# Attention on one core: eight of the fifteen maxima ahead of the first values, and the last output turned later

## The chip, the cores and the metric

The kernel runs on one core of a Trainium2 chip. A core has five engines with instruction queues of their own: TensorE (PE, matrix products, with its weight loads shown apart as PEld), VectorE (DVE), ScalarE (ACT), GpSimd (POOL) and SyncE (SP, which issues transfers). They wait for each other through semaphores alone. The metric is the time of one execution on the device in microseconds (us).

## What is computed

The whole program is an attention, a small mixture of experts on its output, and a two-layer network. The change touches the attention alone, and in it 32 heads (4 batches of 8) that all run through the same steps:

```
batch, n_heads, seq, head_dim = (4, 8, 1152, 64)
q_pool = q.reshape(B, H, S // factor, factor, D).mean(axis=3)      # factor = 2: 576 queries
scores = scale * np.matmul(q_pool, k.transpose(0, 1, 3, 2))        # 576 x 1152
scores = scores - np.max(scores, axis=-1, keepdims=True)
attn = np.exp(scores)
attn = attn / (np.sum(attn, axis=-1, keepdims=True) + 1e-09)
return np.matmul(attn, v).astype(np.float32)
```

## The kernel before

Each head's scores are computed twice. The first time is for the row maxima: 15 pieces of 128 queries by 384 keys, each one matmul (`max_piece` on TensorE, line 382) into one of two PSUM banks and one reduction on VectorE (`max_piece`, line 647). Piece n may be written only when VectorE has reduced piece n-2, since both lie in the same bank; the semaphores `max_freed0` and `max_freed1` say so. I call the pieces maximum 0 to maximum 14. When all fifteen are reduced, one short reduction (line 661) makes the row maximum out of them; it is written into the low part of the queries, which TensorE then turns (`turn_q_lo_m`, line 328 with `q_lo_m`) so that the maximum is subtracted inside the second product.

The second time is for the attention itself, transposed: nine tiles of 128 keys by 576 queries (`score`, two matmuls of line 392 and two of line 401), each followed by an exponential on ScalarE (line 576) into `pT`. Score j needs the exponential of tile j-2, since two tiles' banks alternate. The product with the values (`values`, line 415) goes tile by tile: four tiles in the middle of an iteration, five at its end. GpSimd adds tiles 0 to 6 of the exponentials (line 270), VectorE the last two and the rest (`add_late`, lines 668 to 681), which gives each query's sum.

The loop runs heads in an overlapped way. Iteration h (0 to 30) computes scores, exponentials and values of head h and, between them, the fifteen maxima of head h+1. It also turns the queries of head h+2 (`turn_queries`, line 328 with `q_hi`, four transposes), its keys (`turn_keys`: "ka", "kb" of four transposes each, "kc" of head h+1), and, of head h-1, the finished output (`turn_out`, line 426, three transposes) and its row sums (`sum_rows`, line 431). VectorE's `normalise` (lines 688 to 708, six instructions) then divides that output. Iteration 30 has no head h+2 and leaves those transposes out. The last head, 31, has no maxima beside it; its places are filled with the first steps of the experts.

The order on each engine is written out by hand in this loop; no scheduler moves anything. Engines run their queues strictly in that order. An iteration falls into a first half, from score 0 to the first values, the four tiles of values, a second half from there to `turn_q_lo_m`, and that with the last five tiles of values.

Of the kernel before, what the change touches and what calls it, by code (L numbers as in the profile page):

```python
# [53 lines left out]
def attention(nc, q, k, v, x_all, x_ready, ident, ident_r, ready, ahead):  # L54
# [49 lines left out]
    with ctx:  # L104
# [213 lines left out]
        def _(pe):  # L318
# [12 lines left out]
            def turn_keys(h, name, tiles):  # L331
                if name == "ka":
                    pe.wait_ge(k_split, h + 1)
                claim_turn((name, h))
                sources = [k_parts[h % 2][:, j, :] for j in tiles]
                if name == "kc":
                    sources.append(q_hi2[h % 2][:, QT - 1, :])
                turn_to(turn.bitcast(F32R), sources).then_inc(turned, 1)
# [47 lines left out]
            def score(h, j):  # L386
                u, n = h % 2, h * KT + j
                if n >= 2:
                    pe.wait_ge(exp_done, n - 1)
                out = scores[n % 2]  # L390
                for half in range(2):
                    nc.tensor.matmul(out[:, half, 0:HALF], kT[u][:, j * P:(j + 1) * P],  # L392
                                     qT[h % 3][:, half * HALF:(half + 1) * HALF],
                                     start=True, stop=False)
                if j == 0:
                    pe.wait_ge(k1_copied, h + 1)
                    for use in (Q_LO, Q_LO_LAST):
                        at = max_no(h, use)
                        pe.wait_ge(max_freed[at % 2], at // 2 + 1)
                for half in range(2):  # L400
                    mm = nc.tensor.matmul(out[:, half, 0:HALF], kT1[u][:, j * P:(j + 1) * P],  # L401
                                          qTm[u][:, half * HALF:(half + 1) * HALF],
                                          start=False, stop=True)
                mm.then_inc(scores_ready, 1)

            def values(h, tiles):
                u = h % 2
                if tiles[0] == 0:
                    pe.wait_ge(v_loaded[u], 16 * (h // 2 + 1))
                    pe.wait_ge(qa_copied, min(h + 3, HEADS))  # L410
                for j in tiles:
                    pe.wait_ge(exp_done, h * KT + j + 1)
                    for half in range(2):
                        at = half * SHIFT
                        mm = nc.tensor.matmul(o_bank[half * D:(half + 1) * D, at:at + HALF],  # L415
                                              v_raw[u][:, j, :],
                                              pT[:, j, half * HALF:(half + 1) * HALF],
                                              start=(j == 0), stop=(j == KT - 1))
                    mm.then_inc(pv_done, 1)

            def turn_out(h):

                pe.wait_ge(o_copied, h + 1)
                claim_turn(("out", h))
                for t in range(3):
                    nc.tensor.transpose(turn[:, t * P:(t + 1) * P], oT[:, t * P:(t + 1) * P],
                                        ident[:, :])

            def sum_rows(h):
                pe.wait_ge(groups_summed, h + 1)  # L430
                mm = nc.tensor.matmul(turn[:, 3 * P:3 * P + QT * GROUPS], all_groups[:, :],
                                      group_sums[:, :], start=True, stop=True)
                mm.then_inc(turned, 1)
# [14 lines left out]
            for h in range(HEADS - 1):  # L448
                more2 = h + 2 < HEADS

                def maxima(a, z):
                    for at in range(a, z):
                        max_piece(h + 1, at)

                score(h, 0)
                maxima(0, 2)
                turn_keys(h + 1, "kc", [KT - 1])
                score(h, 1)
                maxima(2, 3)
                score(h, 2)  # L460
                maxima(3, 4)
                if more2:
                    turn_queries(h + 2)
                maxima(4, 5)
                score(h, 3)
                maxima(5, 6)
                if h > 0:
                    turn_out(h - 1)
                maxima(6, 7)
                if h > 0:  # L470
                    sum_rows(h - 1)
                maxima(7, 8)
                score(h, 4)
                maxima(8, 9)
                values(h, range(EARLY))
                maxima(9, 11)
                score(h, 5)
                maxima(11, 12)
                if more2:
                    turn_keys(h + 2, "ka", range(0, 4))  # L480
                maxima(12, 13)
                score(h, 6)
                maxima(13, 14)
                score(h, 7)
                maxima(14, 15)
                score(h, 8)
                if more2:
                    turn_keys(h + 2, "kb", range(4, 8))
                turn_q_lo_m(h + 1)
                values(h, range(EARLY, KT))  # L490
# [6 lines left out]
            first(0, ("x", 1))  # L497
            score(h, 3)
            first(0, ("x", 2))
            turn_out(h - 1)  # L500
            sum_rows(h - 1)
            first(0, ("x", 3))
            score(h, 4)
            first(0, ("x_last",))
            values(h, range(EARLY))
            score(h, 5)
            first(0, ("qk", 0, 0))
# [135 lines left out]
        def _(dve):  # L643
# [90 lines left out]
            maximum(0)  # L734
            for h in range(HEADS - 1):
                for at in range(len(PIECES)):
                    if at == 9 and h > 0:
                        normalise(h - 1)
                    max_piece(h + 1, at)
                maximum(h + 1)  # L740
                add_late(h)

            def add_tile(j, n):

                total, h = p_sum[:, 0:SQ], HEADS - 1
                dve.wait_ge(exp_done, h * KT + j + 1 if j < KT else HEADS * KT)
                if j == KT:
                    dve.wait_ge(part_summed, h * (len(ON_POOL) - 1) + len(LAST_ON_POOL) - 1)
                if n == 0:
                    ins = nc.vector.scalar_tensor_tensor(  # L750
                        total, pT[:, LAST_ON_POOL.stop, :], EPS / P, pT[:, j, :], ALU.add, ALU.add)
                else:
                    dve.wait_ge(p_summed, h * SUM_STEPS + n)
                    ins = nc.vector.tensor_tensor(total, total, pT[:, j, :], ALU.add)
                ins.then_inc(p_summed, 1)
# [2 lines left out]
            first(0, ("x", 0))  # L758
            first(0, ("x", 1))
            first(0, ("x", 2))  # L760
            normalise(h - 1)
            first(0, ("x", 3))
            first(0, ("x_last",))
            add_tile(5, 0)
            first(0, ("qk", 0, 0))
            add_tile(6, 1)
# [1505 lines left out]
```

## Time and profile before

| | us |
|---|---|
| median of 3 runs | 1187.63 |
| lowest, highest | 1186.3, 1188.55 |
| the profiled execution | 1186.41 |
| its span, first to last instruction | 1184.6 |
| TensorE busy | 1122.5 (95%) |
| VectorE busy | 806.1 (68%) |
| GpSimd busy | 673.6 (57%) |
| ScalarE busy | 620.6 (52%) |

The profile comes from one execution. Busy time is the union of an engine's instruction records; a matmul's record includes the pipeline's fill and drain, so that a stretch can show TensorE as fully busy while it issues late. Hence the starts of the records are what to read. The attention's loop takes the first 510 us of the span. Where iterations lie in it:

| stretch, us | iterations |
|---|---|
| 38.16 to 160.76 | 1 to 8 |
| 192.40 to 208.98 | 11 |
| 242.37 to 261.84 | 14 |
| 295.47 to 494.59 | 17 to 29 |
| 494.59 to 509.74 | 30 |

Columns of the busy table by stretch: the stretch and its length; for TensorE, its weight loads, VectorE, ScalarE and GpSimd in that order the us busy and, in brackets, the instructions; the granted TensorE clock as a share of full speed; the DMA engines' busy share; GB/s.

### The profile page before, as it was taken

What the parts mean: (1) busy time and instruction counts of PE and PEld (TensorE: products, weight loads), DVE (VectorE), ACT (ScalarE), POOL (GpSimd) and SP (SyncE); (2) the same over time, 40 slices, a digit from 0 to 9 for tenths busy, and PEclk for the clock granted to TensorE, in tenths of its full rate; (3) what the DMA queues carried; (4) which work ended last, traced back from release to release, by engine and by line L of the source; (5) the groups of instructions that cost most, each with busy time, mean ns of one, the idle gap of its engine ahead of it and who ended that gap; (6) DMA issues with size and microseconds to landing.
All of it is one profiled execution on the core that took longest, in us unless ns stands there. A gap on an engine that the chain in (4) does not pass through costs nothing. (4 is left out here: it accounts for less than half of the span.)

```text
span 1184.6 us, 19899 instructions
## 1 busy us (share of the span) xinstructions
PE 1122.5 (95%) x7088; PEld 930.8 (79%) x7088; DVE 806.1 (68%) x1574; ACT 620.6 (52%) x1228; POOL 673.6 (57%) x687
## 2 busy tenths in 40 slices
PE   6999999989999999998898989789999999999998
PEld 5877777777788777787777777568888898888987
DVE  5888877767888888866556565665448754686554
ACT  4666665566666666655565656632334333443331
POOL 5888899998888888744332335503334333633330
PEclk9999999999999999998999999999999999999999
DMA  8221111211112121001001011123221522223121
GB/s 206 61 61 57 48 53 58 60 43 50 61 61 61 60 61 41 22 1 36 2 1 41 2 38 62 54 87 95 71 72 54 169 64 71 71 64 114 54 71 54
DMA packets 76593, 71.47 MB, mean 60 GB/s; under 512 B 11856, under 2 KB 54864, under 8 KB 76496
## 3 DMA queue, kind: packets, MB, share of 16 engines
q1 hardware_dynamic: 75888, 69.90, 19.7%
q8 instruction: 58, 0.95, 0.3%
q14 instruction: 39, 0.32, 0.1%
q10 hardware_dynamic: 608, 0.30, 0.1%
HBM read 60.74 MB, written 9.44 MB: 59 GB/s over the span
## 5 line engine op out<-in xcount | busy, mean ns | idle before, releaser
L647 DVE TENSOR_REDUCE part_max<-psA 128x1 f32<-128x384 f32 x465 | 250.5, 556 | 60.8 <-PE psA L382 38.0
L576 ACT ACTIVATE pT<-psA 128x576 f32<-128x576 f32 x288 | 187.8, 652 | 164.4 <-PE psA L401 155.1
L270 POOL TENSOR_TENSOR pT<-pT 128x576 f32<-128x576 f32 x157 | 225.3, 1435 | 24.8 <-ACT pT L576 2.8
L382 PE MATMUL psA<-kT,qT 128*128 128x384 f32 x465 | 166.2, 379 | 9.8 <-DVE part_max L647 9.3
L2149 DVE TENSOR_TENSOR hidden_parts<-psC,hidden_parts 128x384 f32<-128x384 f32 x168 | 91.1, 554 | 122.3 <-PE psC L1999 114.9
L415 PE MATMUL psA<-pT,v_raw 128*64 128x288 f32 x1152 | 153.8, 412 | 0.0
L1826 POOL TENSOR_TENSOR w_raw<-w_raw 128x256 f32<-128x256 f32 x24 | 18.3, 762 | 232.3 <-DMA w_raw<-in_moe_w_ch 232.1
L392 PE MATMUL psA<-qT,kT 128*128 128x288 f32 x576 | 132.9, 312 | 0.0
L401 PE MATMUL psA<-qTm,kT 128*128 128x288 f32 x576 | 124.0, 297 | 0.5 <-ACT qTm L562 0.5
L415 PEld LDWEIGHTS psA<-pT,v_raw 128*64 128x64 f32 x1152 | 77.0, 136 | 53.2 <-issue 6.4
L392 PEld LDWEIGHTS psA<-qT,kT 128*128 128x128 f32 x576 | 99.0, 190 | 18.2 <-issue 14.0
L382 PEld LDWEIGHTS psA<-kT,qT 128*128 128x128 f32 x465 | 83.9, 189 | 34.6 <-DVE part_max L647 17.3
L1157 POOL TENSOR_SCALAR moe_probs<-moe_probs,moe_sum_inv,gate 128x128 f32<-128x128 f32 (+4 forms) x80 | 56.3, 704 | 67.4 <-DVE moe_sum_inv L1579 63.2
L401 PEld LDWEIGHTS psA<-qTm,kT 128*128 128x128 f32 x576 | 93.1, 190 | 0.7 <-issue 0.7
L2091 ACT ACTIVATE hid_hi_even<-hidden_parts 128x384 fp32r<-128x384 f32 x48 | 25.3, 526 | 123.4 <-DVE hidden_parts L2149 123.2
L2091 ACT ACTIVATE hid_hi_odd<-hidden_parts 128x384 fp32r<-128x384 f32 x48 | 25.2, 526 | 111.7 <-DVE hidden_parts L2149 111.5
L1999 PE MATMUL psC<-operand,w_hi_even 128*128 128x384 f32 x336 | 75.2, 346 | 5.5 <-DVE w_lo_even L44 4.4
L1440 ACT ACTIVATE moe_probs<-psB,moe_neg_max 128x128 f32<-128x128 f32 (+4 forms) x80 | 45.6, 570 | 65.7 <-DVE moe_neg_max L1592 65.1
L1999 PE MATMUL psC<-operand,w_hi_odd 128*128 128x384 f32 x336 | 73.9, 342 | 4.8 <-DVE x_all L1611 2.7
L1588 DVE COPY_PREDICATED psB<-later,minus 128x128 f32<-128x128 int32 (+1 forms) x80 | 24.0, 300 | 75.8 <-PE psB L1246 75.7
L1999 PEld LDWEIGHTS psC<-operand,w_hi_even 128*128 128x128 f32 x336 | 61.5, 191 | 15.4 <-issue 6.4
L1999 PEld LDWEIGHTS psC<-operand,w_hi_odd 128*128 128x128 f32 x336 | 61.0, 190 | 13.9 <-issue 3.9
(196 smaller groups left out, 2610.3 us busy)
## 6 DMA issues: line engine op xcount, KB each, us to landing
w_raw<-in_moe_w_ch SPq DMA_DIRECT2D x48, 256.0 KB, 3.1
k_raw<-in_k SPq DMA_DIRECT2D x32, 288.0 KB, 2.9
v_raw<-in_v SPq DMA_DIRECT2D x32, 288.0 KB, 2.8
q_raw<-in_q SPq DMA_DIRECT2D x31, 256.0 KB, 3.3
w_even<-in_moe_w_ch SPq DMA_DIRECT2D x12, 512.0 KB, 5.0
w_odd<-in_moe_w_ch SPq DMA_DIRECT2D x12, 512.0 KB, 4.9
u_rows<-x_all SPq DMA_DIRECT2D x16, 256.0 KB, 2.0
u_even<-u_rows SPq DMA_DIRECT2D x2, 1536.0 KB, 7.0
```

The costliest lines, as they stand in the source:

```text
L270: nc.gpsimd.tensor_tensor(pT[:, KT, :], pT[:, KT, :], pT[:, j, :], ALU.add).then_inc(part_summed, 1)
L382: nc.tensor.matmul(maxes[n % 2][:, 0:PIECE], qT[h % 3][:, t * P:(t + 1) * P], kT[u][:, c * PIECE:(c + 1) * PIECE], start=True, stop=True). ...
L392: nc.tensor.matmul(out[:, half, 0:HALF], kT[u][:, j * P:(j + 1) * P], qT[h % 3][:, half * HALF:(half + 1) * HALF], start=True, stop=False)
L401: mm = nc.tensor.matmul(out[:, half, 0:HALF], kT1[u][:, j * P:(j + 1) * P], qTm[u][:, half * HALF:(half + 1) * HALF], start=False, stop=True)
L415: mm = nc.tensor.matmul(o_bank[half * D:(half + 1) * D, at:at + HALF], v_raw[u][:, j, :], pT[:, j, half * HALF:(half + 1) * HALF], start=( ...
L576: nc.scalar.activation(pT[:, j, :].rearrange("p (a c) -> p a c", a=2), scores[n % 2][:, :, 0:HALF], ACT.Exp, scale=0.5 * float(D) ** -0.5) ...
L647: nc.vector.tensor_reduce(part_max[u][:, t, c:c + 1], maxes[n % 2][:, 0:PIECE], AX.X, ALU.max).then_inc(max_freed[n % 2], 1)
L1157: nc.gpsimd.tensor_scalar(p, p, sum_inv[0:rows, e, i:i + 1], gate[b % 2][0:rows, i, e:e + 1], ALU.mult, ALU.mult).then_inc(scaled, 1)
L1440: nc.scalar.activation(probs[n % PROBS][0:rows, 0:width(i)], score_tile(n)[0], ACT.Exp, bias=neg_max[0:rows, e, i:i + 1], accum_out=row_su ...
L1999: mm = nc.tensor.matmul(out[:, 0:W], (hidden.w_hi, hidden.w_lo)[w][n % 2][:, slot - 1, c, :], hidden.part(k, part)[:, c, :], start=(m == 0 ...
L2091: nc.scalar.activation(hidden.hid[0][n % 2][:, b, half * W:(half + 1) * W], quadrants[q], ACT.Relu).then_inc(hid_hi_done, 1)
L2149: nc.vector.tensor_tensor(to, session((k, n))[:, 0:W], other, ALU.add).then_inc(added, 1)
```

## The change

On TensorE, in an iteration: the queries of head h+2 are turned ahead of maximum 3 (before: behind it). Score 4 goes from behind maximum 7 to behind maximum 5. Maxima 6 and 7 follow it, then the output of head h-1 is turned and its rows summed in one go (before: these two stood behind maxima 5 and 6), and the values follow directly. Maximum 8 goes from ahead of the four tiles of values to behind them. In the second half two maxima now stand between values and score 5, two behind it, then the "ka" transposes, score 6, maximum 12, score 7, maxima 13 and 14, and score 8. On VectorE, `normalise` stands ahead of maximum 8 (before: ahead of maximum 9). In the last head, turning, summing and normalising move behind steps ("x", 3), score 4 and ("x_last",) of the experts. No instruction is added or removed; ScalarE, GpSimd and SyncE keep their order.

```diff
--- before.py
+++ after.py
@@ -458,31 +458,27 @@
                 score(h, 1)
                 maxima(2, 3)
                 score(h, 2)
-                maxima(3, 4)
                 if more2:
                     turn_queries(h + 2)
-                maxima(4, 5)
+                maxima(3, 5)
                 score(h, 3)
                 maxima(5, 6)
+                score(h, 4)
+                maxima(6, 8)
+
                 if h > 0:
                     turn_out(h - 1)
-                maxima(6, 7)
-                if h > 0:
                     sum_rows(h - 1)
-                maxima(7, 8)
-                score(h, 4)
-                maxima(8, 9)
                 values(h, range(EARLY))
-                maxima(9, 11)
+                maxima(8, 10)
                 score(h, 5)
-                maxima(11, 12)
+                maxima(10, 12)
                 if more2:
                     turn_keys(h + 2, "ka", range(0, 4))
+                score(h, 6)
                 maxima(12, 13)
-                score(h, 6)
-                maxima(13, 14)
                 score(h, 7)
-                maxima(14, 15)
+                maxima(13, 15)
                 score(h, 8)
                 if more2:
                     turn_keys(h + 2, "kb", range(4, 8))
@@ -497,11 +493,11 @@
             first(0, ("x", 1))
             score(h, 3)
             first(0, ("x", 2))
-            turn_out(h - 1)
-            sum_rows(h - 1)
             first(0, ("x", 3))
             score(h, 4)
             first(0, ("x_last",))
+            turn_out(h - 1)
+            sum_rows(h - 1)
             values(h, range(EARLY))
             score(h, 5)
             first(0, ("qk", 0, 0))
@@ -734,7 +730,7 @@
             maximum(0)
             for h in range(HEADS - 1):
                 for at in range(len(PIECES)):
-                    if at == 9 and h > 0:
+                    if at == 8 and h > 0:
                         normalise(h - 1)
                     max_piece(h + 1, at)
                 maximum(h + 1)
@@ -758,9 +754,9 @@
             first(0, ("x", 0))
             first(0, ("x", 1))
             first(0, ("x", 2))
-            normalise(h - 1)
             first(0, ("x", 3))
             first(0, ("x_last",))
+            normalise(h - 1)
             add_tile(5, 0)
             first(0, ("qk", 0, 0))
             add_tile(6, 1)
```

TensorE, an ordinary iteration, from the transposes of the queries or the maximum behind them to the values. L382 is a maximum, L392 with L401 a score, L328 a transpose, L426 the output turned, L431 the row sums, L415 values. Before:

```order
L382 MATMUL psA<-kT,qT 128x384
L392 MATMUL psA<-qT,kT 128x288 x2
L401 MATMUL psA<-qTm,kT 128x288 x2
L382 MATMUL psA<-kT,qT 128x384
L426 MATMUL psA<-ident,oT 128x128 x3
L382 MATMUL psA<-kT,qT 128x384
L431 MATMUL psA<-group_sums,all_groups 128x20
L382 MATMUL psA<-kT,qT 128x384
L392 MATMUL psA<-qT,kT 128x288 x2
L401 MATMUL psA<-qTm,kT 128x288 x2
L382 MATMUL psA<-kT,qT 128x384
L415 MATMUL psA<-pT,v_raw 64x288 x8
```

Now, the same place:

```order
L328 MATMUL psA<-ident_r,q_hi 128x128 x4
L382 MATMUL psA<-kT,qT 128x384 x2
L392 MATMUL psA<-qT,kT 128x288 x2
L401 MATMUL psA<-qTm,kT 128x288 x2
L382 MATMUL psA<-kT,qT 128x384
L392 MATMUL psA<-qT,kT 128x288 x2
L401 MATMUL psA<-qTm,kT 128x288 x2
L382 MATMUL psA<-kT,qT 128x384 x2
L426 MATMUL psA<-ident,oT 128x128 x3
L431 MATMUL psA<-group_sums,all_groups 128x20
L415 MATMUL psA<-pT,v_raw 64x288 x8
```

Five maxima (4 to 8) stood in the upper piece, five (3 to 7) stand in the lower one; the two short steps on `oT` and `group_sums` have moved from between maxima to the end.

TensorE, the same iteration's second half, from the first maxima behind the values. Before:

```order
L382 MATMUL psA<-kT,qT 128x384 x2
L392 MATMUL psA<-qT,kT 128x288 x2
L401 MATMUL psA<-qTm,kT 128x288 x2
L382 MATMUL psA<-kT,qT 128x384
L328 MATMUL psA<-ident_r,k_parts 128x128 x4
L382 MATMUL psA<-kT,qT 128x384
L392 MATMUL psA<-qT,kT 128x288 x2
L401 MATMUL psA<-qTm,kT 128x288 x2
L382 MATMUL psA<-kT,qT 128x384
L392 MATMUL psA<-qT,kT 128x288 x2
L401 MATMUL psA<-qTm,kT 128x288 x2
L382 MATMUL psA<-kT,qT 128x384
```

Now:

```order
L382 MATMUL psA<-kT,qT 128x384 x2
L392 MATMUL psA<-qT,kT 128x288 x2
L401 MATMUL psA<-qTm,kT 128x288 x2
L382 MATMUL psA<-kT,qT 128x384 x2
L328 MATMUL psA<-ident_r,k_parts 128x128 x4
L392 MATMUL psA<-qT,kT 128x288 x2
L401 MATMUL psA<-qTm,kT 128x288 x2
L382 MATMUL psA<-kT,qT 128x384
L392 MATMUL psA<-qT,kT 128x288 x2
L401 MATMUL psA<-qTm,kT 128x288 x2
L382 MATMUL psA<-kT,qT 128x384 x2
```

Six maxima before, seven now; two pairs of them now stand with nothing between.

## Rows read from the trace of the kernel before

**Rows 1.** By engine: stretch, length, us busy (instructions), granted clock, DMA share, GB/s.
```profile
38.16:160.76 122.60, 122.49 (x890) 97.24 (x888) 101.27 (x209) 81.46 (x152) 103.11 (x84) 1.00 0.20 59
...
192.40:208.98 16.58, 15.52 (x114) 12.14 (x112) 12.92 (x27) 10.19 (x19) 15.78 (x15) 1.00 0.18 54
...
242.37:261.84 19.47, 17.05 (x114) 13.53 (x112) 13.32 (x27) 10.29 (x19) 18.67 (x16) 0.91 0.16 46
...
295.47:494.59 199.12, 198.94 (x1446) 157.86 (x1444) 164.03 (x339) 131.15 (x245) 163.56 (x129) 1.00 0.17 53
494.59:509.74 15.15, 14.84 (x101) 11.10 (x99) 12.30 (x27) 7.41 (x14) 11.91 (x17) 1.00 0.07 21
```

**Rows 2.** Timeline, TensorE, iteration 18: start, length, line, what, count, idle before.
```profile
310.78 0.53 PE L392 MATMUL psA<-qT,kT 128*128 128x288 f32 x2
...
313.21 0.35 PE L382 MATMUL psA<-kT,qT 128*128 128x384 f32 x1
313.39 0.46 PE L328 MATMUL psA<-ident_r,q_hi 128*128 128x128 f32 x4
313.69 0.41 PE L382 MATMUL psA<-kT,qT 128*128 128x384 f32 x1
313.94 0.42 PE L392 MATMUL psA<-qT,kT 128*128 128x288 f32 x2
...
314.47 0.34 PE L382 MATMUL psA<-kT,qT 128*128 128x384 f32 x1
...
315.46 0.44 PE L382 MATMUL psA<-kT,qT 128*128 128x384 f32 x1
...
316.53 2.16 PE L415 MATMUL psA<-pT,v_raw 128*64 128x288 f32 x16
318.62 0.62 PE L382 MATMUL psA<-kT,qT 128*128 128x384 f32 x2
319.08 0.42 PE L392 MATMUL psA<-qT,kT 128*128 128x288 f32 x2
...
319.72 0.45 PE L382 MATMUL psA<-kT,qT 128*128 128x384 f32 x1
320.00 0.46 PE L328 MATMUL psA<-ident_r,k_parts 128*128 128x128 f32 x4
...
323.01 0.59 PE L328 MATMUL psA<-ident_r,q_lo_m 128*128 128x128 f32 x5
```

**Rows 3.** Timeline, VectorE, same iteration: four single maxima, then the overall maximum.
```profile
313.60 0.56 DVE L647 TENSOR_REDUCE part_max<-psA 128x1 f32<-128x384 f32 x1 [0.16 <-PE psA L382]
...
319.10 0.56 DVE L647 TENSOR_REDUCE part_max<-psA 128x1 f32<-128x384 f32 x1 [0.68 <-PE psA L382]
...
319.58 0.55 DVE L647 TENSOR_REDUCE part_max<-psA 128x1 f32<-128x384 f32 x1
...
322.14 0.56 DVE L647 TENSOR_REDUCE part_max<-psA 128x1 f32<-128x384 f32 x1
322.74 0.17 DVE L661 TENSOR_REDUCE q_lo_m<-part_max 128x5 fp32r<-128x15 f32 x1
```

**Rows 4.** Timeline, TensorE, last head: turned output, row sums, next matmul.
```profile
513.53 0.49 PE L426 MATMUL psA<-ident,oT 128*128 128x128 f32 x3
...
514.07 0.65 PE L1303 MATMUL psB<-ident,x_all 128*128 128x128 f32 x4
```

**Rows 5.** Timeline, TensorE, second half of iteration 30.
```profile
503.43 0.90 PE L382 MATMUL psA<-kT,qT 128*128 128x384 f32 x2
...
506.65 0.59 PE L328 MATMUL psA<-ident_r,q_lo_m 128*128 128x128 f32 x5 [0.25 <-issue]
```

**Rows 6.** Waits, 20 to 505 us: us in total, times, longest.
```profile
DVE p_sum L673 <- POOL pT L270: 10.7, 7, 2.9
...
PE psA L382 <- DVE part_max L647: 9.3, 8, 2.4
```

**Rows 7.** Busy time inside iteration 14, columns as above.
```profile
248.00:250.00 2.00, 2.00 (x11) 1.90 (x10) 1.11 (x2) 1.25 (x2) 2.00 (x3) 0.50 0.07 5
```

## The prediction

> **What bounds the kernel now.** I read the busy time by stretch first, to see whether the loop is regular. Iterations 1 to 8 and 17 to 29 are: 122.60 / 8 = 15.33 us and 199.12 / 13 = 15.32 us each [rows 1]. Iterations 10 to 16 are longer, as iteration 11 with 16.58 us and 14 with 19.47 us, and there GpSimd is busy 15.78 of 16.58 us [rows 1]: it also splits the experts' weights. The waits say what that does: VectorE waits seven times for GpSimd's sums, 10.7 us in all, the longest 2.9 [rows 6].
>
> In the regular iterations TensorE looks fully busy, 198.94 of 199.12 us [rows 1]. The second thing to see is that this is not so. Iteration 30 has no head h+2 to turn, twelve transposes less; four take about 0.3 us (313.39 to 313.69) [rows 2], so it should be some 0.9 us shorter. It is 15.15 us, 0.17 shorter [rows 1]. Something else paces TensorE: the ring of the maxima, which is read from the two timelines. A maximum's matmul that had to wait lasts 0.45 us (319.72), one that did not 0.35 (313.21) [rows 2], and the reduction starts 0.04 behind its end (313.60) [rows 3]. The reduction takes 0.56 (319.10 to 319.66) [rows 3], and the next matmul into that bank starts 0.06 later, at 319.72 [rows 2]. So one bank turns round in 0.45 + 0.04 + 0.56 + 0.06 = 1.11 us, and one bank serves every second maximum. VectorE is quicker by itself: a reduction that is ready ends 0.47 behind the one ahead of it (319.66 to 320.13) [rows 3]. At the end of the second half stands a hard gate: the last reduction ends at 322.70, the overall maximum starts at 322.74 [rows 3], and TensorE turns the low queries at 323.01 [rows 2], 0.31 behind the last reduction.
>
> **The prices for walking through the new order** [rows 2]: a score takes 0.53 (313.94 to 314.47), a maximum 0.18 (313.21 to 313.39), 0.28 if it waited (319.72 to 320.00) or stands first behind values, 0.25 behind transposes (313.69 to 313.94), four transposes 0.30. Output turned plus row sums: 0.54 (513.53 to 514.07) [rows 4].
>
> **The first half.** Before, the values start 316.53 - 310.78 = 5.75 us behind score 0, and maximum 3 at 2.43 [rows 2]; up to there nothing changes. Now the queries' transposes stand there, and maximum 3 comes at 2.73, its reduction ends at 2.73 + 0.41 + 0.04 + 0.56 = 3.74. Maximum 4 at 2.98, score 3 from 3.16 to 3.69. Maximum 5 waits for reduction 3 until 3.80; score 4 from 4.08 to 4.61; maximum 6 at 4.61; maximum 7 waits for reduction 5 (3.80 + 1.05 = 4.85) until 4.91; 0.28 and 0.54 later, at 5.73, the values start. One maximum has gone from the half and 0.02 us is won: the gap beside reductions 5 to 7 swallows it. Without any wait in it the half would take 5.2 us (the same steps added up, 0.11 of waits at 5, 0.12 at 7, two restarts of 0.1, and the last-head price for turning and summing perhaps 0.1 to 0.2 too high). So the first half gives between 0.02 and 0.55 us; I take 0.02 since every wait in it follows from rows of this loop.
>
> The values take the same 2.09 us (316.53 to 318.62) [rows 2]. `normalise` is hidden behind them as before: VectorE then still idles 0.68 us until TensorE's next maximum (row 319.10) [rows 3]. If that cover were gone, up to 1.3 us per iteration would show, but it starts earlier now, not later, since reduction 8 has gone from ahead of it.
>
> **The second half, where the cost is.** Time runs from its first maximum. Before: 323.01 - 318.62 = 4.39 us to the turn of the low queries [rows 2]. Now maximum 8 at 0, its reduction from 0.48 to 1.04; maximum 9 at 0.28, its reduction ends at 1.51; score 5 from 0.46 to 0.99; maximum 10 waits for reduction 8 until 1.10, its reduction ends at 2.15; maximum 11 waits for reduction 9 until 1.57; then 0.28, "ka" until 2.15, score 6 until 2.68. Only there stands maximum 12, whose bank has been free since 2.21. Reduction 12 ends at 2.68 + 0.35 + 0.04 + 0.56 = 3.63; score 7 ends at 3.39; maximum 13 there, its reduction ends at 4.34; maximum 14 waits until 3.69, and its reduction would start at 4.18 but VectorE is at 13 until 4.34, so it ends at 4.81. With 0.31 for the gate the low queries are turned at 5.12 us. That is 0.73 later than before. TensorE reaches the gate with score 8 and "kb" at about 4.80 and stands still for 0.3 us. Bounds from rows: the four reductions of one bank alone need 3 x 1.11 + 0.48 + 0.56 + 0.31 = 4.68 (+0.29); with every score after a transpose 0.07 slower it is 5.19 (+0.80).
>
> The sum of an ordinary iteration is 0.73 - 0.02 = +0.71 us, I take +0.70; with the ends of both halves it lies between -0.26 and +0.78, the low end only if every wait of the first half vanishes and every hold of the second too. Nearest to the rows is the upper part, +0.3 to +0.78.
>
> **How many iterations.** Iterations 0 to 7 and 17 to 29 pay it, and 16 too, whose start GpSimd releases but whose second half is ordinary: 22. In between GpSimd has hardly a break (15.78 of 16.58 us busy in iteration 11) [rows 1], and VectorE waits for it seven times; leaving out the longest, (10.7 - 2.9) / 6 = 1.3 us each [rows 6]. The first of these, at the end of iteration 9, is filled by the 1.4 us that iterations 8 and 9 add; from 10 to 15 GpSimd's work alone makes an iteration longer than the 15.33 + 0.70 = 16.03 us that TensorE will need (16.58 in iteration 11, 19.47 in 14) [rows 1], so nothing is added. If GpSimd's cover fails, 7 x 0.7 = 4.9 more. Iteration 30 has no transposes, so that its reductions run earlier: in the second half it already waits for two maxima in a row (503.43, two records in 0.90 us) and has idle time ahead of the low queries (0.25 us by row 506.65) [rows 5]; I give it +0.2. The last head's move costs 0: TensorE has the same instructions, and VectorE's division stands in idle time; 0.3 either way.
>
> The sum: 22 x 0.70 + 0.2 = 15.6 us. Against the profiled execution's own 1186.4 this is 1202.0 us; the three runs' median lies 1.2 higher (1187.6), and from it I forecast **1203 us**. ScalarE and GpSimd add nothing of their own: in these iterations ScalarE is busy 131.15 / 13 = 10.1 and GpSimd 163.56 / 13 = 12.6 of 15.3 us [rows 1], so both wait for TensorE. VectorE's sums behind exponential 8 move with score 8 and still lie beside the five tiles of values.
>
> **The rivals.** (1) *TensorE is the pace of the second half after all.* If a bank turned round within the work that stands between (under about 0.9 us instead of 1.11), the second half would grow only by the seventh maximum, 0.18, of which the stand ahead of the gate (0.1) hides a part, while the first half gives 0.3 of its waits: -0.22 x 22 = -5, **1183 us**, faster. For it speaks that TensorE's records fill 99.9% of the stretch [rows 1]; against it the 1.11 us read directly and iteration 30, which lost twelve transposes and won 0.17.
>
> (2) *A draw.* If the first half gives all of its 0.55 and the second costs 0.5 to 0.6, little is left: 1186 to 1190.
>
> (3) *The clock falls.* In iteration 14, behind the longest wait, the granted clock fell, to 0.50 of full speed (the lower level, 1.2 of 2.4 GHz) in the stretch 248 to 250 us [rows 7]; that iteration shows 17.05 us of TensorE busy for the work that takes 15.52 in iteration 11, whose waits of about 1.3 us on VectorE left the clock at 1.00 [rows 1]. The new waits are 0.1 to 0.3 us each. If they did it nevertheless, 1.5 us on each of 22 iterations would add 33: about 1236 us. The Trainium skill has such a case ("TensorE: Matmul & The Clock Gate", A second HAM failure mode: psum-queue depth-cycling): a kernel that cycles through PSUM banks lets TensorE idle in small pieces often enough to swing between the two clock levels. This kernel cycles through two banks fifteen times per head already at a granted clock of 1.00, so by this trace the rule does not bite at this size of wait.
>
> (4) *GpSimd's iterations pay as well*: 1203 + 5 = 1208.
>
> **How the numbers follow.** Forecast with (4) and the lower prices of the second half, all slower: 0.85 (of that 0.07 for (4)). Faster (1): 0.07. Draw (2): 0.05. Clock (3): 0.03. The bound for faster, same and slower is 0.2%, 2.4 us, about what a measurement of this kernel can tell from no change. So faster 0.07, same 0.05, slower 0.88. For the range: 22 x 0.35 + 0.2 = 8 gives 1195.5 at the low end; 22 x 0.78 + 4.9 = 22 gives 1209.5 at the high end. I take 1195 to 1210, which leaves about 0.18 outside.
>
> **What would show it.** Regular iterations of 16.0 us instead of 15.3; first half 5.7 (before 5.75), second half 5.1 (before 4.39); TensorE's idle or late start ahead of the low queries 0.3 us; a wait at maxima 10, 11 and 14; iterations 10 to 15 as long as before, and the seven waits for GpSimd fewer and shorter at the first of them. The forecast is wrong if the second half stays below 4.7, if the first half falls to 5.3, or if the clock of the regular stretch leaves 1.00.

## The result, and the profile after

| | before | changed |
|---|---|---|
| median of 4 runs, us | 1186.97 | 1203.85 |
| lowest, highest | 1186.14, 1188.55 | 1202.45, 1206.53 |
| ratio, 95% interval | | 1.0136 (1.0121 to 1.0151) |
| the profiled execution | 1186.41 | 1206.53 |

The change makes the kernel 1.4% slower; 1203 us was forecast. The changed kernel's page gives these busy times:

```profile
PE 1141.6 (95%) x7088; PEld 935.4 (78%) x7088; DVE 794.3 (66%) x1574; ACT 620.2 (51%) x1228; POOL 672.4 (56%) x687
```

TensorE's busy share is 95% in both, and GpSimd's and ScalarE's busy times hardly differ; VectorE's is 11.8 us lower. TensorE's is 19.1 us higher, 1141.6 against 1122.5, although it has the same instructions: a table of busy times counts late starts as work, and does not tell a slower kernel's waits from its work. The busy time by stretch tells where the loss is; it is for iterations 1 to 8, 11, 14, 17 to 29 and 30 of the changed kernel, with the columns of [rows 1]:

```profile
38.85:167.10 128.25, 126.82 (x891) 98.00 (x889) 97.56 (x209) 81.31 (x152) 103.74 (x84) 1.00 0.19 56
199.18:215.65 16.47, 16.09 (x113) 12.26 (x111) 12.03 (x26) 10.17 (x19) 15.67 (x15) 1.00 0.19 55
249.28:267.13 17.85, 16.08 (x113) 12.26 (x112) 13.38 (x26) 10.17 (x19) 17.05 (x15) 1.00 0.18 50
301.19:509.70 208.51, 206.18 (x1445) 159.40 (x1444) 157.97 (x339) 130.98 (x245) 163.41 (x129) 1.00 0.17 51
509.70:525.05 15.35, 14.83 (x101) 11.10 (x100) 12.14 (x27) 7.40 (x14) 12.38 (x17) 1.00 0.07 21
```

Iterations 17 to 29 take 208.51 / 13 = 16.04 us (before 15.32 [rows 1]); 1 to 8 take 16.03 (before 15.33); iteration 30 takes 15.35 (before 15.15). Iteration 11, where GpSimd sets the time, is as long as before (16.47 against 16.58). Iteration 14 has even become shorter, 17.85 against 19.47, with the granted clock at 1.00 instead of 0.91; the next one has become longer, so that iterations 9 to 16 take 134.1 us in all against 134.7.

TensorE's timeline of iteration 18 answers to [rows 2] (start, length, what, count, idle before):

```profile
317.21 0.53 PE L392 MATMUL psA<-qT,kT 128*128 128x288 f32 x2
...
319.94 0.59 PE L382 MATMUL psA<-kT,qT 128*128 128x384 f32 x2
...
321.00 0.44 PE L382 MATMUL psA<-kT,qT 128*128 128x384 f32 x1
...
321.81 0.73 PE L382 MATMUL psA<-kT,qT 128*128 128x384 f32 x2
322.38 0.49 PE L426 MATMUL psA<-ident,oT 128*128 128x128 f32 x3
322.70 0.30 PE L431 MATMUL psA<-group_sums,all_groups 128*128 128x20 f32 x2
322.93 2.16 PE L415 MATMUL psA<-pT,v_raw 128*64 128x288 f32 x16
325.02 0.62 PE L382 MATMUL psA<-kT,qT 128*128 128x384 f32 x2
...
326.11 0.91 PE L382 MATMUL psA<-kT,qT 128*128 128x384 f32 x2
326.86 0.46 PE L328 MATMUL psA<-ident_r,k_parts 128*128 128x128 f32 x4
327.15 0.50 PE L392 MATMUL psA<-qT,kT 128*128 128x288 f32 x2
...
327.76 0.33 PE L382 MATMUL psA<-kT,qT 128*128 128x384 f32 x1
...
328.46 0.73 PE L382 MATMUL psA<-kT,qT 128*128 128x384 f32 x2
329.03 0.43 PE L392 MATMUL psA<-qT,kT 128*128 128x288 f32 x2
...
329.56 0.45 PE L328 MATMUL psA<-ident_r,k_parts 128*128 128x128 f32 x4
330.16 0.60 PE L328 MATMUL psA<-ident_r,q_lo_m 128*128 128x128 f32 x5
```

The starts, counted from score 0 at 317.21: maximum 3 at 2.73, maximum 5 at 3.79, values at 5.72 (the row 322.93), maximum 8 at 7.81. From maximum 8 at 325.02: maximum 10 at 1.09, the keys' transposes at 1.84, score 6 at 2.13, maximum 12 at 2.74, maxima 13 and 14 from 3.44, the low queries at 5.14. Before, the second half took 4.39. VectorE's reductions of the same second half, and the overall maximum:

```profile
325.50 2.12 DVE L643 TENSOR_REDUCE part_max<-psA 128x1 f32<-128x384 f32 x4 [1.07 <-PE psA L382]
328.13 1.72 DVE L643 TENSOR_REDUCE part_max<-psA 128x1 f32<-128x384 f32 x3 [0.52 <-PE psA L382]
329.89 0.17 DVE L657 TENSOR_REDUCE q_lo_m<-part_max 128x5 fp32r<-128x15 f32 x1
```

Four reductions in 2.12 us run almost without a break, then VectorE is idle 0.52 us: maximum 12 stands behind score 6, although its bank has been free for 0.6 us. The last reduction ends at 329.85 and the low queries are turned 0.31 later. What waited for what, over all iterations (us in total, times, longest):

```profile
DVE part_max L643 <- PE psA L382: 86.1, 143, 2.3
...
PEld psA L382 <- DVE part_max L643: 38.9, 159, 1.9
...
DVE p_sum L669 <- POOL pT L270: 5.2, 4, 1.3
```

The first two of these in the kernel before:

```profile
DVE part_max L647 <- PE psA L382: 38.0, 91, 2.8
PEld psA L382 <- DVE part_max L647: 17.3, 41, 2.6
```

TensorE's weight loads ahead of a maximum waited 159 times and 38.9 us for reductions. Before, these were 41 waits and 17.3 us; VectorE waited 38.0 us for maxima, now 86.1. Both sides of the ring wait more: the two wait in turn. TensorE's matmuls themselves show no more idle time for reductions than before (4.5 us in 5 waits, before 9.3 in 8 [rows 6]); the wait is seen at the weight loads and in the late starts. VectorE's waits for GpSimd's sums have fallen from 7 to 4 and from 10.7 us [rows 6] to 5.2.

### The profile page after: what moved, and what is told of

It is laid out like the page before. It is cut to its first block and busy times, and to the rows that moved or that the text cites. A ratio compares the mean times of both kernels' runs of the same rounds, so it can differ in the third digit from the quotient of the medians.

```text
span 1204.7 us, 19899 instructions
## 1 busy us (share of the span) xinstructions
PE 1141.6 (95%) x7088; PEld 935.4 (78%) x7088; DVE 794.3 (66%) x1574; ACT 620.2 (51%) x1228; POOL 672.4 (56%) x687
## 5 line engine op out<-in xcount | busy, mean ns | idle before, releaser
L643 DVE TENSOR_REDUCE part_max<-psA 128x1 f32<-128x384 f32 x465 | 241.9, 553 | 98.1 <-PE psA L382 86.1
L382 PE MATMUL psA<-kT,qT 128*128 128x384 f32 x465 | 161.8, 388 | 5.2 <-DVE part_max L643 4.5
L415 PE MATMUL psA<-pT,v_raw 128*64 128x288 f32 x1152 | 153.9, 412 | 0.0
L392 PE MATMUL psA<-qT,kT 128*128 128x288 f32 x576 | 131.4, 310 | 0.0
L401 PE MATMUL psA<-qTm,kT 128*128 128x288 f32 x576 | 123.2, 296 | 0.5 <-ACT qTm L558 0.5
L382 PEld LDWEIGHTS psA<-kT,qT 128*128 128x128 f32 x465 | 80.8, 188 | 52.8 <-DVE part_max L643 38.9
L415 PEld LDWEIGHTS psA<-pT,v_raw 128*64 128x64 f32 x1152 | 77.0, 137 | 47.8 <-issue 0.2
L392 PEld LDWEIGHTS psA<-qT,kT 128*128 128x128 f32 x576 | 98.6, 189 | 14.0 <-issue 14.0
L401 PEld LDWEIGHTS psA<-qTm,kT 128*128 128x128 f32 x576 | 92.6, 189 | 0.7 <-issue 0.7
L237 POOL TENSOR_TENSOR k_parts<-k_raw,k_parts 128x576 fp32r<-128x576 f32 x31 | 44.1, 1424 | 59.2 <-ACT k_parts L526 59.1
```

What stands on the lines that cost most here:

```text
L382: nc.tensor.matmul(maxes[n % 2][:, 0:PIECE], qT[h % 3][:, t * P:(t + 1) * P], kT[u][:, c * PIECE:(c + 1) * PIECE], start=True, stop=True). ...
L643: nc.vector.tensor_reduce(part_max[u][:, t, c:c + 1], maxes[n % 2][:, 0:PIECE], AX.X, ALU.max).then_inc(max_freed[n % 2], 1)
```

## Experiments

In the tables, "first half" is from score 0 to the values, "second half" from the first maximum behind the values to the turn of the low queries, medians over the ordinary iterations of one trace. The ratio is to the kernel before on the same chip. In each, VectorE's division stands ahead of the first maximum behind the values. In the diffs, words in brackets stand for lines left out.

| kernel | first half | second half | iteration | ratio (95%) |
|---|---|---|---|---|
| before | 5.75 | 4.39 | 15.32 | |
| changed | 5.70 | 5.14 | 16.03 | 1.0136 (1.0121 to 1.0151) |
| only the turned output moved | 6.20 | 4.39 | 15.78 | 1.0068 (1.0048 to 1.0087) |
| only maximum 8 moved | 5.56 | 5.14 | 15.89 | 1.0094 (1.0077 to 1.0111) |
| changed, seven in front | 5.31 | 5.53 | 16.04 | 1.0130 (1.0115 to 1.0145) |
| before, ten in front | 6.13 | 3.97 | 15.29 | 0.9998 (0.9984 to 1.0012) |
| changed, old order of scores 6, 7 | 5.72 | 4.94 | 15.85 | 1.0110 (1.0072 to 1.0148) |
| before, half reductions | 5.55 | 4.08 | 14.82 | 0.9927 (0.9900 to 0.9953) |
| changed, half reductions | 5.30 | 4.35 | 14.84 | 0.9906 (0.9874 to 0.9938) |
| changed, half behind the values | 5.72 | 4.35 | 15.25 | 0.9993 (0.9973 to 1.0013) |
| changed, half in front | 5.29 | 5.14 | 15.62 | 1.0045 (1.0026 to 1.0065) |
| before, keys early | 5.73 | 4.42 | 15.34 | 1.0003 (0.9987 to 1.0019) |

**The two parts of the change, each alone.** First the turned output alone, on the kernel before:

```diff
-                maxima(5, 6)
+                maxima(5, 8)
+                score(h, 4)
+                maxima(8, 9)
                 if h > 0:
                     turn_out(h - 1)
-                maxima(6, 7)
                 if h > 0:
                     sum_rows(h - 1)
-                maxima(7, 8)
-                score(h, 4)
-                maxima(8, 9)
                 values(h, range(EARLY))
```

> The kernel before with one part of the change: the last output is turned and its rows summed directly ahead of the values, all nine maxima stay in front. Theory (ring of two banks, 1.11 us a turn, plus the gate ahead of the low queries): the two short steps had filled time in which maxima 6 and 7 waited for their banks. Without them maximum 6 waits until 3.98, maximum 7 until 4.70, score 4 ends at 5.51, and with maximum 8 and 0.54 the values start at 6.2 us instead of 5.75; second half unchanged at 4.39. Ordinary iteration 15.8 us instead of 15.32, in all 22 x 0.48 = +10.6: about 1197.5 us. Rival (the move of these steps is free, all of the loss is the second half's): 15.32, 1187 us.

The median was 1196.25 us, 1.0068 of the kernel before; an ordinary iteration 15.78. In the timeline of iteration 18 (it begins at 314.42):

```profile
318.08 0.72 PE L382 MATMUL psA<-kT,qT 128*128 128x384 f32 x2
319.07 0.44 PE L382 MATMUL psA<-kT,qT 128*128 128x384 f32 x1 [0.27 <-DVE part_max L645]
...
320.62 0.71 PE L415 MATMUL psA<-pT,v_raw 128*64 128x288 f32 x4
```

Maxima 5 and 6 are the first row; maximum 7 waits: TensorE is idle 0.27 us until 319.07, 4.65 from the start (4.70 expected). The values begin at 6.20. The rival falls: this move is not free, because the two short steps had filled waits.

Then maximum 8 alone, with the second half of the changed kernel:

```diff
                 score(h, 4)
-                maxima(8, 9)
                 values(h, range(EARLY))
-                maxima(9, 11)
+                maxima(8, 10)
                 score(h, 5)
-                maxima(11, 12)
+                maxima(10, 12)
                 (keys)
-                maxima(12, 13)
                 score(h, 6)
-                maxima(13, 14)
+                maxima(12, 13)
                 score(h, 7)
-                maxima(14, 15)
+                maxima(13, 15)
```

> The kernel before with the other part alone: maximum 8 behind the values, the second half as in the changed kernel, the first half as before without maximum 8 (output turned and rows summed between maxima 5, 6 and 7 as before). Theory: first half 5.75 - 0.27 = 5.48, second half 5.12 instead of 4.39; ordinary iteration 15.8 us, +0.47, in all +10.3: about 1197.3 us. Rival (the loss of the change is the place of the turned output): first half 0.27 shorter, second half 0.2 longer by the matmul alone: 15.3 us, 1186.

1200.32 us, 1.0094. Iterations 17 to 29 (columns as in [rows 1]):

```profile
300.44:506.94 206.50, 203.89 (x1446) 158.57 (x1444) 159.50 (x339) 131.01 (x245) 163.37 (x129) 1.00 0.17 51
```

206.50 / 13 = 15.88 us. The second half is the changed kernel's to the hundredth (5.14), the first 5.56 instead of the 5.48 expected, which over 22 iterations is 1.8 of the 3 us by which the median misses the 1197.3 expected. The rival, which put the loss on the turned output, falls as well. The parts do not add up (0.46 + 0.57 = 1.03 against 0.71 of both together): in the changed kernel the first half has one maximum less and score 4 between maxima 5 and 6, so it should miss the two short steps less; that is my reading and no run of its own.

**More and fewer maxima in front.** Seven in front, on the changed kernel:

```diff
-                maxima(6, 8)
+                maxima(6, 7)
                 (output turned, rows summed, values)
-                maxima(8, 10)
+                maxima(7, 9)
                 score(h, 5)
-                maxima(10, 12)
+                maxima(9, 11)
                 (keys)
                 score(h, 6)
-                maxima(12, 13)
+                maxima(11, 13)
```

> The changed kernel with one more maximum behind the values: seven in front, eight behind. Theory: in front maximum 7's wait (0.12), its restart (0.10) and its own 0.18 go, so the values start at 5.33; behind, the ring holds maxima 9, 10, 13 and 14 and the low queries are turned at 5.57 instead of 5.12. Ordinary iteration 16.1 us against 16.03 of the changed kernel: 1204 to 1206 us. Rival (every maximum that goes behind the values costs the 0.7 us that the first one did): 16.7 us, about 1219.

```profile
301.21:509.63 208.42, 206.77 (x1445) 159.92 (x1443) 158.04 (x339) 131.01 (x245) 163.50 (x129) 1.00 0.17 51
```

208.42 / 13 = 16.03 us, the changed kernel's own; the median 1204.42. The first half is 0.39 us shorter, the second 0.39 longer. A rule "a maximum behind the values costs 0.7", which the change itself suggests, is 15 us off here, and the walk through the ring is not. Then ten in front, on the kernel before:

```diff
-                maxima(8, 9)
+                maxima(8, 10)
                 values(h, range(EARLY))
-                maxima(9, 11)
+                maxima(10, 11)
                 (score 5, maximum 11, keys, maximum 12, score 6)
-                maxima(13, 14)
+                maxima(13, 15)
                 score(h, 7)
-                maxima(14, 15)
```

> The other direction from the kernel before: ten maxima in front, five behind; maximum 14 directly behind 13, ahead of score 7; the division ahead of maximum 10. Theory: maximum 9 waits little (its bank comes free at 5.77, the values would start at 5.75), so the first half is 0.3 to 0.4 longer; the second half falls from 4.39 to 4.0, where TensorE's own work ends it. Ordinary iteration 15.2 to 15.3 us, 1184 to 1187. Rival (VectorE's amount of work behind the values alone sets the time): 0.7 us less per iteration, 1172.

1188.39 us, 0.9998: no change. The iteration is inside the 15.2 to 15.3 us expected, the time 1.4 us above the 1187. The rival, 1172 us, falls: 0.42 us less behind the values was paid with 0.38 in front. Iterations 1, 16 and 17 to 29:

```profile
37.02:54.38 17.36, 15.51 (x113) 12.06 (x111) 14.63 (x29) 9.92 (x19) 13.32 (x11) 1.00 0.18 53
278.76:297.57 18.81, 17.01 (x113) 13.49 (x112) 14.59 (x29) 10.04 (x19) 13.26 (x11) 0.91 0.16 48
297.57:496.21 198.64, 198.44 (x1446) 156.66 (x1444) 161.70 (x339) 127.82 (x245) 163.54 (x129) 1.00 0.18 53
```

The ordinary iteration has gained 0.04 us (198.64 / 13 = 15.28). Iteration 1 takes 17.36 us (before 15.30), of which iteration 0 gives 1.41 back (16.14, before 17.55), and 16 takes 18.81 (before 17.19) at a granted clock of 0.91; that eats the gain. In iteration 1 maximum 2 waits 1.84 us for VectorE, which waits for GpSimd's sums; why only in this order was not followed up.

**The order within the second half**, on the changed kernel:

```diff
                 (keys)
-                score(h, 6)
                 maxima(12, 13)
+                score(h, 6)
+                maxima(13, 14)
                 score(h, 7)
-                maxima(13, 15)
+                maxima(14, 15)
```

> The changed kernel with the second half's last maxima in the old places: maximum 12 ahead of score 6, 13 ahead of score 7, 14 ahead of score 8. Theory: maximum 12 no longer stands behind score 6 with its bank free; its matmul starts at 2.21 instead of 2.74, maximum 14 at 3.73 without a wait, the low queries at 4.99 instead of 5.14. Ordinary iteration 15.9 us, 0.13 to 0.15 less: about 1200.5 us. Rival (the number of maxima behind the values is all that counts): as the changed kernel, 1203.9.

```profile
298.85:504.80 205.95, 205.65 (x1446) 160.16 (x1444) 159.19 (x339) 131.20 (x245) 163.62 (x129) 1.00 0.17 51
```

205.95 / 13 = 15.84 us; the second half is 4.94 instead of 5.14 (4.99 expected). In time 1201.43 us (1200.5 expected), 1.0110 with a wide interval (1.0072 to 1.0148), which does not by itself part it from the changed kernel; the iterations do. With seven maxima behind the values in both, their number is not all that counts.

**Quicker reductions.** In `max_piece` on VectorE (the kernel leaves half of the keys out of the row maxima):

```diff
-  part_max[u][:, t, c:c + 1], maxes[n % 2][:, 0:PIECE],
+  part_max[u][:, t, c:c + 1], maxes[n % 2][:, 0:PIECE // 2],
```

On the changed kernel:

> The changed kernel with each of the fifteen reductions reading only half of its 384 columns (half of the keys is left out of the row maxima), matmuls as they are. Theory: a bank turns round in 0.9 us instead of 1.11 and no matmul waits; first half 5.2 to 5.3, second half 4.2, ordinary iteration 14.6 to 14.7 us; iterations 10 to 16 are GpSimd's and hardly move: 1203.9 - 22 x 1.35 = 1172 to 1175 us. Rival (the loss is TensorE's own: restarts and kinds of matmul that follow each other): the iteration stays 0.7 us above that of the kernel before with the same half reductions.

```profile
289.67:482.54 192.87, 192.87 (x1446) 158.84 (x1444) 127.93 (x340) 131.06 (x245) 166.24 (x129) 1.00 0.19 55
```

and on the kernel before:

> The kernel before with each of the fifteen reductions reading only half of its 384 columns (half of the keys is left out of the row maxima). Theory: first half 5.5, second half 4.05, ordinary iteration 14.7 us, within 0.1 of the changed kernel with the same half reductions: 1172 to 1175 us, so the change's 17 us shrink to within 3. Rival (TensorE is the pace before and VectorE is not on its path): stays 15.3 us, 1187.

```profile
289.95:482.50 192.55, 192.55 (x1444) 156.03 (x1444) 130.03 (x340) 129.44 (x246) 166.05 (x129) 1.00 0.19 55
```

192.87 / 13 = 14.84 and 192.55 / 13 = 14.81 us: the difference of 0.71 has gone to 0.03, TensorE's busy time is the whole stretch in both, and the medians are 1177.18 and 1178.86 (1172 to 1175 expected for both). The rivals, which put the loss or the pace on TensorE's own work, fall. The changed kernel's iteration is 0.15 longer than expected. TensorE's timeline of its second half, and the overall maximum on VectorE, show why:

```profile
311.88 0.62 PE L382 MATMUL psA<-kT,qT 128*128 128x384 f32 x2
...
312.86 0.62 PE L382 MATMUL psA<-kT,qT 128*128 128x384 f32 x2
313.31 0.46 PE L328 MATMUL psA<-ident_r,k_parts 128*128 128x128 f32 x4
...
315.80 0.46 PE L328 MATMUL psA<-ident_r,k_parts 128*128 128x128 f32 x4
316.22 0.58 PE L328 MATMUL psA<-ident_r,q_lo_m 128*128 128x128 f32 x5
```

```profile
315.95 0.17 DVE L657 TENSOR_REDUCE q_lo_m<-part_max 128x5 fp32r<-128x15 f32 x1
```

The low queries come 4.34 us behind maximum 8 (316.22 - 311.88), where 4.2 had been worked out. The last four transposes would be through at 316.10 (315.80 and 0.30), which is 4.22. But the overall maximum ends only at 316.12, and the low queries follow it by 0.10: the gate still holds TensorE for 0.12 us. So even with half reductions not every wait is gone.

The kernel before has a hold of its own that is not the ring's. Score 8 needs exponential 6; here are that exponential and score 8's first matmul in iteration 18:

```profile
321.26 0.65 ACT L576 ACTIVATE pT<-psA 128x576 f32<-128x576 f32 x1 [0.17 <-PE psA L401]
...
321.97 0.40 PE L392 MATMUL psA<-qT,kT 128*128 128x288 f32 x1
```

The exponential ends at 321.91 and the matmul starts 0.06 later, with the longer record of one that waited; this score takes 0.62 us (to 322.59) instead of 0.53. With half reductions it is the same there (0.05 behind its exponential). In the changed kernel the exponential is done well before score 8.

These two runs split the loss. With half reductions the two halves take 5.55 + 4.08 = 9.63 us before and 5.30 + 4.35 = 9.65 after: the change moved about 0.26 us from one half to the other. That is TensorE's own work and the 0.1 to 0.2 us of holds just named. What halving takes away is waits for reductions: before 0.20 and 0.31, after 0.40 and 0.79. So the waits that the reductions' length sets have grown by 0.68 us, 0.20 of it in front and 0.48 behind, which is nearly all of the loss of 0.71.

The same, for one half at a time, on the changed kernel (the condition is `at >= 8`, then `at < 8`; those parts of the maxima leave out half of their keys):

```diff
-  maxes[n % 2][:, 0:PIECE],
+  maxes[n % 2][:, 0:PIECE // 2 if at >= 8 else PIECE],
```

> The changed kernel, only the reductions of maxima 8 to 14 read half of their columns (half of the keys is left out of those parts of the row maxima). Theory (the waits behind the values are the larger part): second half 4.35 as with all reductions halved, first half 5.70 as in the changed kernel; ordinary iteration 15.25 us, below the kernel before (15.32); 1186 to 1188 us. Rival (the loss is in front of the values): nothing moves, 16.0 us, 1204.

```profile
296.02:494.27 198.25, 198.25 (x1446) 159.20 (x1444) 142.95 (x339) 131.07 (x245) 163.44 (x129) 1.00 0.18 53
```

> The changed kernel, only the reductions of maxima 0 to 7 read half of their columns (half of the keys is left out of those parts of the row maxima). Theory: first half 5.30, second half 5.14; ordinary iteration 15.63 us; 1195 us. Rival (the loss is in front of the values): 15.2 us or less, 1186.

```profile
295.31:498.40 203.09, 200.64 (x1445) 158.89 (x1443) 139.77 (x339) 131.06 (x245) 163.62 (x129) 1.00 0.17 52
```

198.25 / 13 = 15.25 and 203.09 / 13 = 15.62 us, as expected to 0.01. Freed of the waits behind the values the changed kernel is as quick as the kernel before with its own waits (0.9993); freed of those in front it is still 1.0045. The medians are 1187.13 us (1186 to 1188 expected) and 1192.68 (1195 expected; iteration 0 took 16.05 us there and not 17.79).

**The last head**, changed alone on the kernel before (its lines of the diff for heads below 31 undone):

> The kernel before with the change of the last head alone (turning, summing and dividing head 30's output behind the experts' first steps). Last head from its score 0 to the end of its first stretch: 7.92 us before, 8.52 in the changed kernel. If the order in the last head does it: 8.5 us here; if it is only what the iteration ahead leaves: 7.9. The time is within 1 us of the kernel before either way.

One run, 1188.21 us: as said, the time could not show it. The last head takes 8.52 us from its score 0 to score 5, as in the changed kernel, against 7.92. TensorE, last head of this kernel:

```profile
513.88 0.66 PE L1303 MATMUL psB<-ident,x_all 128*128 128x128 f32 x4 [0.38 <-DVE xT_lo L44]
...
515.38 0.55 PE L426 MATMUL psA<-ident,oT 128*128 128x128 f32 x3
```

The transposes of ("x", 3) wait 0.38 us for VectorE's line 44. Before, the output was turned and its rows summed just there [rows 4], in the time of this wait. Here they start at 515.38 and the values 0.61 later, at 515.99.

**An attempt to better the kernel before**, with the keys' transposes where maximum 11 waited:

```diff
                 score(h, 5)
-                maxima(11, 12)
                 if more2:
                     turn_keys(h + 2, "ka", range(0, 4))
-                maxima(12, 13)
+                maxima(11, 13)
                 score(h, 6)
-                maxima(13, 14)
+                maxima(13, 15)
                 score(h, 7)
-                maxima(14, 15)
```

> The kernel before with other fillings of the second half: the keys' transposes directly behind score 5, where maximum 11 waits for its bank, then maxima 11 and 12, score 6, maxima 13 and 14, and score 7 behind 14, so that two scores and the last transposes cover the way from the last maximum to the low queries. Theory: second half 4.31 instead of 4.39, set by TensorE's own work and no longer by the gate; ordinary iteration 15.24 us, 22 x 0.08 = 1.8 us less: about 1187 against 1188.9 of the kernel before on these chips, hardly to be told by the time but by the iterations. Rival (the gate is all that counts in the second half): 4.1, 0.3 us less per iteration, 6 us in all.

```profile
296.05:495.53 199.48, 199.01 (x1446) 157.77 (x1444) 160.03 (x339) 127.91 (x245) 163.63 (x129) 1.00 0.18 53
```

It failed: 199.48 / 13 = 15.34 us, second half 4.42. The wait of maximum 11 has gone, but maximum 14 directly behind 13 waits for 12's reduction instead, and the late restart behind that wait costs as much. The rival, which wanted 0.3 less, is wrong too. No kernel here that computes the whole result beats the kernel before.

## Why the prediction was right, and where it was off

**Pace.** That the ring of two banks and the gate ahead of the low queries hold TensorE, although its records fill the stretch, was shown by the half reductions: 0.50 us of each iteration before, 1.19 after, go with them. Halving alone does not part the ring from a VectorE that is simply too slow. For that there are the starts: in the changed kernel maximum 10 (326.11) starts 0.05 behind the end of reduction 8 (325.50 and 0.56), and VectorE then stands idle 0.52 us within that same half. No run gave the maxima a third bank. What the pace account left out is ScalarE, of which the prediction said that it adds nothing: in the kernel before, score 8 waits for exponential 6.

**First half.** Forecast 5.73, measured 5.70 to 5.72; the waits at maxima 5 and 7 stand where they were worked out (3.79 against 3.80, 4.88 against 4.91).

**Second half.** Forecast 5.12, measured 5.14. Two small errors nearly cancel: score 6 behind the transposes takes 0.61 instead of 0.53, near the price that the upper bound had, so that it ends at 2.74 and not 2.68; from there to the low queries it is 2.40 us and not 2.44.

**Iterations.** Forecast 22 that pay 0.70 and one that pays 0.2. Measured: 1 to 8 grew by 5.65 us, 9 to 16 shrank by 0.62, 17 to 29 grew by 9.39, iteration 30 by 0.20, and 0 and what lies ahead of it by 0.69: 15.3 against 15.6. The total is nearer than its parts. Iteration 0 itself grew by 0.24 only; 0.45 lies ahead of it, where the change touches nothing (in the thirteen traces iteration 0 begins between 20.3 and 21.1 us). Iteration 16, counted as paying 0.70, became 1.06 shorter, and 15, counted as unchanged, 1.47 longer. That these came out even in sum is luck. What I had not seen is that the long wait of iteration 14 would be shared out between two iterations (2.40 us before; 1.60 and 1.64 now) and the clock there stay up.

**The last head** was the term that was mis-sized: forecast 0, at most 0.3, measured 0.60, and the run that changed it alone gave the same 0.60. The step that failed was "TensorE has the same instructions": I priced the move by its work, while in the loop I had counted what waits it filled. The same mechanism, missed once.

**The rivals.** TensorE as the pace of the second half: excluded by the half reductions. The draw: excluded, since the first half gave 0.05 us and not 0.55. The falling clock: 1.00 in all ordinary iterations of the changed kernel, whose late starts are 0.1 to 0.3 us; by this trace such waits did not lower it. GpSimd's iterations did not pay in sum.

**The whole.** The loop and the last head lose 15.9 us by the traces (the last head's score 5 starts at 533.57 instead of 517.66). The rest of the program, which the change does not touch, took 666.95 us in the profiled execution before and 671.18 in the changed one; over the profiled executions of all these kernels it lies between 666.2 and 672.3, and the half-reduction kernels, which have the same code there, gave 666.9 and 672.0. So these 4 us are one execution's scatter and not the change's; of the measured 16.9 us between the medians 15.9 are found in the traces, 15.5 of them where the change can act (without the 0.45 ahead of iteration 0), and both lie within the interval (14.4 to 17.9).

## What to carry to other kernels

Where two engines pass work through two buffers, read the turn of one buffer (write, hand over, read, hand back) and compare it with the other work between its two uses: work taken out of a stretch where the ring waits can gain next to nothing (here 0.05 us), and a step put into one that is already short costs more than its own length (here 0.75 us, 0.20 of it through the order, for a matmul that is followed after 0.18). A short step that stands beside a wait is free there and has its full price elsewhere, often more than its own length. Busy shares do not tell of it; halve the suspected reader's work and see whether the difference between two versions goes.

## What was not expected of the hardware

A wait costs TensorE more than the time waited: a maximum that waited was followed 0.28 us later by the next matmul (319.72 to 320.00 [rows 2]), one that did not after 0.18. VectorE's reductions end 0.47 us apart when the next one is ready, although each record is 0.55 to 0.56 long (319.10 and 319.58 [rows 3]).

TensorE's clock did not go by the length of one idle stretch. Behind iteration 14's longest one, 2.40 us, the granted clock was 0.50 before the change [rows 7], while the changed kernel, with more but shorter waits (the longest 1.60 and 1.64 us), kept 1.00 from iteration 1 to 30. But with half reductions the changed kernel had an idle stretch of 2.82 us and went on at 1.00 (the first two lines), and with half reductions behind the values alone one of 1.66 us was followed by 0.50 (the last two):

```profile
242.17 0.45 PE L382 MATMUL psA<-kT,qT 128*128 128x384 f32 x1 [2.82 <-DVE part_max L643]
242.20:246.00 3.80, 3.80 (x29) 3.73 (x31) 2.16 (x8) 2.44 (x4) 3.80 (x4) 1.00 0.10 11
...
281.19 0.44 PE L382 MATMUL psA<-kT,qT 128*128 128x384 f32 x1 [1.66 <-DVE part_max L643]
282.00:285.00 3.00, 3.00 (x15) 2.99 (x14) 1.25 (x3) 1.43 (x3) 2.48 (x2) 0.50 0.02 5
```

So the clock that the changed kernel kept in iteration 14 is not safely the change's doing, and what decides it stays open.
